# A wait on a TensorE step ahead of each scatter, in a kernel whose order a small planner writes

## The reference

```python
sig = 1.0 / (1.0 + np.exp(-f_logit))
f = lower_bound + (1.0 - lower_bound) * sig
for t in range(S):
    h = f[:, t] * h + (1.0 - f[:, t]) * x[:, t]
    y[:, t] = h
...
logits = xn @ en.T / tau              # rows and expert vectors at length 1
expert_idx = np.argmax(logits, axis=1)
gate_w = probs[np.arange(N), expert_idx]
for e in range(E):
    mask = expert_idx == e
    h = np.maximum(x[mask] @ w1[e], 0.0)          # 256 -> 1024
    out[mask] = gate_w[mask, None] * (h @ w2[e])  # 1024 -> 256
```

## Time and profile before

| what | us |
|---|---|
| median of 3 runs (lowest to highest) | 658.78 (655.96 to 660.06) |
| the profiled execution, whole | 658.78 |
| its span, first instruction to last | 657.0 |
| PE busy | 527.1 (80% of the span) |
| POOL busy | 365.5 (56%) |
| DVE, ACT busy | 384.7, 341.2 |
| 324 scatters on POOL (L1011, L1268) | 166.1 + 168.8 |
| data moved | 94.83 MB, mean 144 GB/s |

### The profile page before, as it was taken

How to read it: one execution, slowest core, us unless ns; L and a number is a source line. 1 busy time by engine, 2 the same in 40 slices (tenths; PEclk the granted TensorE clock), 3 DMA queues, 4 the chain that set the end, 5 groups by cost and what they waited for, 6 DMA issues and landing times.

```text
span 657.0 us, 14749 instructions
## 1 busy us (share of the span) xinstructions
PE 527.1 (80%) x4139; PEld 445.5 (68%) x4139; DVE 384.7 (59%) x1120; ACT 341.2 (52%) x850; POOL 365.5 (56%) x462
## 2 busy tenths in 40 slices
PE   5686658789888697898888886977878899889991
PEld 5565547568767485786776765765767788778780
DVE  6796759568665676677665765764334344444440
ACT  7868775567465465576555464632323244333340
POOL 4255865567555554665646455554544546655563
PEclk9898976899879888899898798897978999999996
DMA  8999699576444364565545432224433335433300
GB/s 307 276 283 317 210 216 267 126 201 174 144 135 135 114 183 138 163 187 140 168 153 136 145 102 59 71 70 126 111 86 91 98 97 106 101 96 97 84 28 31
DMA packets 97050, 94.83 MB, mean 144 GB/s; under 512 B 75012, under 2 KB 77071, under 8 KB 96976
## 3 DMA queue, kind: packets, MB, share of 16 engines
q1 hardware_dynamic: 81584, 53.61, 31.1%
q0 software_dynamic: 15392, 40.27, 21.1%
HBM read 58.38 MB, written 34.01 MB: 141 GB/s over the span
## 4 chain that ended last, share of the span: by engine, by line
PE 51%; issue 17%; POOL 8%; DVE 8%; another core or an unknown queue 7%; ACT 5%; DMA 3%; POOLq 0%; ACTq 0%; DVEq 0%; SPq 0%
PE bank L1213 17%; PE bank L1245 15%; POOL out_dram L1268 6%; PE bank L680 5%; PE bank L753 5%; PE bank L713 4%; DVE hb L736 3%; DMA fin<-in_f_logit_dram 3%; PE bank L821 2%; PE bank L838 2%; DVE nx L720 2%; POOL pace L472 2%; ACT fg L696 1%; ACT fg L690 1%
## 5 line engine op out<-in xcount | busy, mean ns | idle before, releaser
L1268 POOL DMA_INDIRECT out_dram<-osb,xm x166 | 168.8, 1017 | 166.3 <-DVE osb L1263 48.1
L1245 PE MATMUL bank<-w2b,hT 128*128 x1328 | 195.2, 283 | 36.7 <-issue 18.4
L1213 PE MATMUL bank<-ys,w1b 128*128 128x256 bf16 x1328 | 203.8, 290 | 20.7 <-issue 15.7
L1011 POOL DMA_INDIRECT XsScratch<-Yt,sli x158 | 166.1, 1051 | 64.4 <-issue 44.8
L1234 DVE TENSOR_SCALAR hT<-bank 128x512 bf16<-128x512 f32 x166 | 112.7, 685 | 137.9 <-PE bank L1213 67.1
L1213 PEld LDWEIGHTS bank<-ys,w1b 128*128 x1328 | 162.3, 146 | 43.5 <-issue 36.8
L1245 PEld LDWEIGHTS bank<-w2b,hT 128*128 128x128 bf16 x1328 | 129.0, 102 | 67.3 <-issue 50.7
L1229 ACT ACTIVATE hT<-bank 128x512 bf16<-128x512 f32 x166 | 97.6, 599 | 148.0 <-PE bank L1213 90.5
L736 DVE TENSOR_TENSOR_SCAN hb<-fg,hb,nx 128x512 f32<-128x512 f32 (+4 forms) x78 | 96.6, 1243 | 0.5
L690 ACT ACTIVATE fg<-bank 128x512 f32<-128x512 f32 (+1 forms) x80 | 46.2, 600 | 77.9 <-PE bank L680 26.9
L680 PE MATMUL bank<-ident,fin 128*128 128x128 f32 x316 | 56.6, 320 | 33.8 <-DMA fin<-in_f_logit_dram 9.7
(11 more groups left out here) (115 smaller groups left out, 336.8 us busy)
## 6 DMA issues: line engine op xcount, KB each, us to landing
fin<-in_f_logit_dram SPq DMA_DIRECT2D x39, 512.0 KB
xin<-in_x_dram SPq DMA_DIRECT2D x39, 512.0 KB
w1b<-in_moe_w_dram POOLq DMA_DIRECT2D x8, 512.0 KB, 10.5
w2b<-in_moe_w_dram POOLq DMA_DIRECT2D x8, 512.0 KB, 11.3
out_dram<-osb,xm POOLq DMA_INDIRECT x166
XsScratch<-Yt,sli POOLq DMA_INDIRECT x158
ys<-XsScratch SPq DMA_TRANSPOSE x83
xm<-XsScratch SPq DMA_DIRECT2D x83, 2.0 KB
```

Of the source, the lines that this page charges most:

```text
L1011: lambda e, j=o + j, i=o + k_ * 4 + b: e.indirect_dma_start(out=Xs[:, :], out_offset=bass.IndirectOffsetOnAxis(ap=sli[y][:, j : j + 1], axis=0
L1213: i = e.matmul(bank[h.b][:, fi * T : (fi + 1) * T], wb[0][:, bass.ds(w0, P, step=FT)], ys[qy][:, kt, :], start=(kt == 0), stop=(kt == DT - 1),
L1245: i = e.matmul(po(s), hT[qh][:, kf, s * P : (s + 1) * P], wb[1][:, bass.ds(evr[j] + kf * D, D)], start=(kf == 0 and s == 0), stop=(kf == F ...
L1268: lambda e, s=s: e.indirect_dma_start(out=out[:, :], out_offset=bass.IndirectOffsetOnAxis(ap=xm[qx][:, s, 1:2], axis=0), in_=osb[qo][:, s, :],
```

## The change

After the planning and before the waits are made, the program goes once through the planned order. It keeps a list of the PE steps whose end some other engine reads. For each POOL DMA of less than 500000 bytes (the scatters and two small fills of `XsScratch` at the start, but not the 512 KB weight loads of L661) it looks at the last 40 of these steps, takes the latest one that the plan ends at least 1800 ns ahead of the DMA's planned start, and adds it to what the DMA waits for. The planned order itself stays.

```diff
         pr.total = pr.schedule(clear, {"a": 5, "m": 6, "o": 2})
+
+
+        read = {id(d) for o in pr.out if o.eng != "pe" for d in o.deps}
+        done = []
+        for o in pr.out:
+            if o.eng == "pe" and id(o) in read and not o.part:
+                done.append(o)
+            elif o.eng == "pool" and o.dma is not None and o.nbytes < 500000 and not o.part:
+                early = [x for x in done[-40:] if x.start + x.cost <= o.start - 1800]
+                if early:
+                    o.deps.append(early[-1])
         block = es.enter_context(nc.Block())
```

## The result

| what | before | after |
|---|---|---|
| median (lowest to highest), 4 runs of each | 659.3 (655.96 to 660.06) | 603.87 (601.89 to 604.64) |
| ratio, 95% interval | | 0.9164 (0.9124 to 0.9203) |
| the profiled execution, its span | 658.78, 657.0 | 601.89, 600.1 |
| mean granted clock of PE over the span | 0.909 | 0.956 |

A forecast was written before the change was run, and what follows sets the result against it. The prediction took PE to idle because rows of back-to-back POOL scatters hold its increments. From 658.8 us it took 29.3 (middle), 5.7 (last tiles) and 2 (start), giving 622 us, range 597 to 657.

The forecast's parts named there:

- What bounds the kernel: While POOL issues scatters back to back, PE's `s_pe` increments reach other engines only some 0.65 us after the row ends.
- Rows shrink to two or three; no more rows of five to ten: POOL's rows of scatters: each new wait finds its step held, so POOL stops after about two or three scatters.
- long rows still there: Sign in the timeline that the prediction is wrong: rows of five to ten scatters 0.30 us apart remain.
- The price, 1.66 us a scatter: POOL's queue: a pair with a break costs 3.32 us, 1.66 a scatter in place of 1.33; lateness taken as hidden.
- The middle, -29.3 us: 129 to 526 us: long rows' stretches reach the short rows' 89.7% busy PE, 257.1 us in place of 286.40.
- near 90%: Sign of being right: PE's busy share from 130 to 526 us, with near 100% in the last tiles.
- The last tiles, -5.7 us: 526 to 639 us: rows of four reach 99.7% busy PE, 80.4 us in place of 86.10.
- The start, -2 us: To 129 us: a 6.08 us hold shortened gives -4, breaks among eight scatters cost 2; ends -4 and +2.
- The clock, left out of the sum: Rival, chance 0.22: PE's clock comes back too, 20 us more from half-rate time, giving 602 us.
- The "remote" waits under a third: Sign of being right: ACT's and DVE's "remote" waits ahead of PSUM work fall from 100.8 us to under a third.
- No gain: Rival, chance 0.10: holds change shape, not sum; the middle keeps its 67 us idle, about 655 us.
- POOL as the bound: Rival, chance 0.13: in POOL's queue every scatter waits out a hold, 1.98 us each, 694 us.

The follow-up runs named there:

- run 1: The changed kernel with only the scatters to `XsScratch` and the two fills waiting for a PE step: 615.92 us, 0.9267 of the kernel before.
- run 2: The changed kernel with only the 166 scatters to `out` waiting for a PE step: 640.83 us, 0.9642 of the kernel before.
- run 3: Pauses by pairs: the kernel before, no added waits, with eight short POOL instructions after every second small DMA: 622.1 us, ratio 0.9339.
- run 5: The kernel before, no added waits, with sixteen short POOL instructions after every fourth small DMA: 621.57 us, ratio 0.9483.
- the runs with 3600: The changed kernel with 3600 ns in place of 1800 between PE step and scatter in the plan: 617.0 us, 0.9411 of the kernel before.
- waits and pauses together: The changed kernel with four short POOL instructions after every second small DMA as well: 606.43 us, 0.925 of the kernel before.
- a distance of 0: The changed kernel with 0 ns in place of 1800 between PE step and scatter in the plan: 606.96 us, 0.915 of the kernel before.
- the mixed run: Third chip: pauses after every second small DMA planned before 220 us, the change's waits after that: 577.99 us, 1.0694 of the kernel before.
- the kernel with 7200: Third chip: the changed kernel with 7200 ns between PE step and scatter, last 80 steps looked at: 538.94 us, 0.9963 of the kernel before.

## Why the prediction was right, and where it was not

*What bounds the kernel.* Right, as far as the runs go: back-to-back scatters go with held PE increments. Taking the scatters to `out` away gives 15.3%; keeping all and breaking their rows by pauses gives 4.8 of the last tiles' 6.4 us and 20.3 to 28.8 of the middle's 44.7; and the same order of work takes 540 us on a chip where increments are not held. A hold shows in the earlier trace rows as "remote", and it still shows in the kernel after. The picture of a hold was too simple, as it was read from one row of seven. Over all 29 rows of five or more in the kernel before, 149 increments are recorded while a row is under way, against 319 steps that end in one; and the first increment behind a row comes 0.07 to 1.48 us after its end, 1.15 in the median, not 0.65.

*Rows shrink to two or three; no more rows of five to ten.* This step failed, and "long rows still there" is one of the prediction's own signs of being wrong. 19 rows of five or more with 128 scatters are left. The prediction took each scatter's step as one that is still held until POOL stops. In the trace many steps have been seen when POOL comes to their scatter, as in the five scatters at 424.83, with increments that pass in the middle of the row. That a POOL late against its plan finds its steps long done is a likely reason for the rest, but the planned times are in no trace.

*The price, 1.66 us a scatter.* Nothing measures it as forecast. From the first scatter to the last there are now 547.4 us for 324, 1.69 each, but that is the pace of the program (1.877 before), and its nearness is luck: POOL's waits that a PE step ends stand ahead of about a quarter of the scatters, not half. In the three rows above they are 52.9 us in 48 waits, 1.10 us each, where the sum took 0.65 + 0.30. POOL's lateness stayed hidden, as taken: no row of `osb` waiting for a scatter's DMA stands in the list of waits.

*The middle, -29.3 us.* In PE's idle time 25.3 us went, close to the term. That is in part luck, as the way there was another one: not all stretches at 89.7%, but long rows fewer and less harmful (85.3%), and PE busy 87.0% of the whole middle, not "near 90%".

*The last tiles, -5.7 us.* 6.4 us, at PE busy 106.19 of 106.90 us, 99.3%. Runs 1, 2, 3 and 5 show that it is the length of the rows of `out` that decides here.

*The start, -2 us.* 5.9 us, outside its ends of -4 and +2. Runs 1 and 2 show that the waits do it (96.0 us with those of `XsScratch`, 101.2 without). The clock rose there too (0.88 to 0.91), but PE's busy time fell by only 1.3 us, so 4.6 us are idle time; the term was sized by one hold on the chain, and others beside it were left out.

*The clock, left out of the sum.* This is the mis-sized step: nothing was taken, and 19.4 us came in the middle alone, in a row that holds the same matmuls at 0.97 in place of 0.90. The rival put it at 20 us. It was left out because one stretch with idle PE stood at 1.00; the price was right and the chance too low. The prediction's own mark for it, a clock above 0.95 from first scatter to last, is met (0.97). Worked as it did from the earlier trace rows, the time at 1.2 GHz fell from 97 us to 2 x 0.03 x 547 = 33. The Trainium skill (TensorE: Matmul & The Clock Gate, "HAM oscillation — how this bites in real kernels") says that idle gaps of PE throw its clock back. The rows of the pauses by pairs agree, with 1.00 in steps 200 to 400, where PE idles 5.6 of 103.90 us, and 0.84 in steps 600 to 700, where it idles 19.4 of 76.40; but the change stands at 1.00 in steps 600 to 700 with 10.2 us of 58.70 idle, so the idle share alone does not tell the clock.

*The "remote" waits under a third.* Missed by a little: 39.2 of 100.8 us, where a third is 33.6.

*The rivals.* No gain fell by the result. POOL as the bound did not come with the waits and did come with pauses, at the place named, `osb`. The Trainium skill (Trainium Architecture — The Big Picture, "What this means for kernel authors") says that engines do not block one another without a semaphore. On the first chips the runs contradict it, with the 0.9339 of pauses that hold POOL alone and move the same bytes; on the third chip the traces agree with it.

*Open.* How the middle's gain divides between shorter rows and a POOL kept near PE: steps 200 to 400 speak for the first, the runs with 3600 and with waits and pauses together for the second. The number of long holds does not order the runs either: steps held over 2.5 us are 67 before and 53 after, 64 with a distance of 0 (0.915) and 24 with pauses by pairs (0.9339). Why increments are held on some chips and not on another wasn't found, and no run was made for it: the chip, and what runs beside it, are not in a trace.

## What to carry to other kernels

When consumers of one engine wait for a "remote" on a single core, look at what another engine issues at that time, and compare the same step beside few and beside many of these issues. Pace such an issuer by a wait for the progress of the engine that it disturbs rather than by fixed pauses: a wait that is already met cost nothing (0.999), while pauses made the issuer the bound where its work is dense (17.7 us lost to the change in steps 600 to 700, and 1.0694 in the mixed run, where there was nothing to cure). And when PE's idle gaps shrink, price its clock with them: here that was 19 us beside 25.

## What was not expected of the hardware

- The same kernel takes 540.37 us on one chip and 656.71 to 667.44 on others, 22 to 24% more, with the mean granted clock of its runs at 0.955 to 0.966 on the first and 0.894 to 0.922 on the others. The traces differ in the held increments, 16 of 718 against 366 of 707 (the first in the kernel with 7200, as the kernel before left no trace there). Single instructions are no faster there: a scatter takes 1041 and 1091 ns (1017 and 1051 in the earlier trace rows), `hT` 598 and 685 ns (599 and 685).
- Holds did not get rarer with the change, 486 held increments where there were 366, and it still gained 8.4%: so it seems to count whether PE has work queued that doesn't need them. In the middle, 39.8 of PE's 75.4 idle us lay inside holds before, 25.6 of 50.1 after; inside holds of over 2.5 us it was 26.8 and 12.6.
- On the chip without holds, plain POOL DMAs in place of indirect ones still give 2.7% (0.9726); POOL's busy time there is 297.3 us against 375.3 with 7200.
